# Float32 matmuls in attention and in the product of two weights, heads on row and column halves

## The chip, the cores and the metric

The kernel runs on one core of a Trainium2 chip. The metric is the device time of one execution in microseconds. TensorE (PE) multiplies, VectorE (DVE), ScalarE (ACT) and GpSimd (POOL) compute element by element, SyncE (SP) issues the DMAs. Each engine runs its own instruction stream in order; semaphores order the engines among each other. PEld is the loading of the stationary operand, which overlaps PE.

## The reference

All inputs are float32. Attention over a window of 128 keys, then two gated layers:

```python
batch, n_heads, seq, head_dim = (4, 8, 576, 64)
scores = scale * np.matmul(q, k.transpose(0, 1, 3, 2))
scores = np.where(mask, scores + bias[None], -1000000000.0)   # mask: 0 <= query - key < 128
...
x = np.matmul(attn, v)                    # softmax(scores) @ v, reshaped to 2304 x 512
gate = 1.0 / (1.0 + np.exp(-(x @ w_gate)))
x = gate * (x @ w_val) @ w_out            # 512 -> 1536 -> 512
a = x @ w1
b = x @ w2
h = a * b @ w3                            # 512 -> 1024 -> 1024
out = h @ w_out2                          # -> 512
```

## The kernel before

Every matmul is made of float32r operands. A value is held as a high part (its float32r cast, made on ScalarE) and a low part (value minus high part, on VectorE or POOL), and a product is three matmuls: high x high, high x low, low x high (`product`, L592 to L597). Since `a * b @ w3 @ w_out2` is linear in its last two weights, the kernel multiplies w3 by w_out2 itself, once: 64 products of 128x128 by 128x512 (`fold`, L653), stored to memory and loaded back as the output weight of the second layer.

The tokens go in three passes of 768. A pass has ten groups g of hidden columns, six of the first layer and four of the second. For a group there is a "gate" and a "val" section, each seven products of a fast 2x2 scheme with 384 tokens each (42 matmuls, `multiply`, L675), and mostly a "proj" section (48 matmuls, `project`, L710; "pair0" and "pair1" at the end of a layer). POOL and ScalarE split each group's weights (`weight_sums`, `plain_lo`, `sums_lo`, `out_lo`, L1282 to L1322; `weights_hi`, `out_hi`); VectorE and ScalarE evaluate the results (`keep`, `gate`, `hidden`, `add_up`). At a change of layer the new x is split (`x_hi`, `x_sum`, `x_lo`). Results of a pass stand in `xf` and are stored by `store_pass` (L516), one DMA.

Attention has 80 steps of 128 queries for two heads, grouped in 32 jobs of two or three steps which share loaded keys, queries and values. The keys of a step are one or two chunks of 128 (16 steps have one), 144 chunks in all. A step is: `scores` (L599: head h on rows 64h to 64h+63 of the array, six matmuls), `score` on VectorE (bias, minimum), `exponentials` on ScalarE, `reciprocals` on VectorE, `normalise` on POOL, `turn` on PE (float32 transposes, L622), `turned_hi` on ScalarE and `turned_lo` on VectorE, `pv` on PE (L637, three matmuls a chunk, each 128 columns of values of both heads by 256 columns of probabilities of both heads; the two quarters that pair one head's values with its own probabilities are used) and `out_copy` on ScalarE (L816), one copy per head. Keys, queries and values are split by `keys_hi`, `queries_hi`, `values_hi` (ACT, L769 to L792) and `keys_lo`, `queries_lo`, `values_lo` (POOL, L1232 to L1257).

The first 28 steps (`HEAD`) run ahead of the passes in slots (L730), with lags of 3 to 8 slots between the parts of a step (L69) and two folds per slot; 52 steps run inside the sections of passes 0 and 1, one per section, in the order written for each engine. The PE order in a section is: scores of step n, then the section's products with `turn` of step n-1 after the second and `pv` after the fifth. `scores` waits for the low parts (L603, L604). Two buffer sets for keys, queries and values serve the passes, three the head (`set_of`, L154).

## Time and profile before

| | |
|---|---|
| median of 3 runs | 1037.02 us (1035.7 to 1039.22) |
| profiled execution | 1036.08 us, span 1034.2 us |
| PE busy | 932.4 us, 90% of the span, 5352 matmuls |
| PEld busy | 867.3 us, 84% |
| POOL busy | 736.5 us, 71% |
| ACT busy | 562.4 us, 54% |
| DVE busy | 559.1 us, 54% |
| mean granted PE clock | 0.957 |
| DMA | 80.79 MB, 23.9% of the 16 engines' time |

Busy time of PE counts from the start of a matmul to its modelled end; matmuls overlap, so the distance between two starts, not the duration, is what one costs in a dense stream.

### The profile page before, as it was taken

What the parts mean: (1) busy time and instruction counts of PE and PEld (TensorE: products, weight loads), DVE (VectorE), ACT (ScalarE), POOL (GpSimd) and SP (SyncE); (2) the same over time, 40 slices, a digit from 0 to 9 for tenths busy, and PEclk for the clock granted to TensorE, in tenths of its full rate; (3) what the DMA queues carried; (4) which work ended last, traced back from release to release, by engine and by line L of the source; (5) the groups of instructions that cost most, each with busy time, mean ns of one, the idle gap of its engine ahead of it and who ended that gap; (6) DMA issues with size and microseconds to landing.
All of it is one profiled execution on the core that took longest, in us unless ns stands there. A gap on an engine that the chain in (4) does not pass through costs nothing. (4 is left out here: it accounts for less than half of the span.)

```text
span 1034.2 us, 16072 instructions
## 1 busy us (share of the span) xinstructions
PE 932.4 (90%) x5352; PEld 867.3 (84%) x5352; DVE 559.1 (54%) x1280; ACT 562.4 (54%) x1295; POOL 736.5 (71%) x627
## 2 busy tenths in 40 slices
PE   3988787999997989977999998879987999998998
PEld 2766677999996879976999997869887999997998
DVE  5435353566655556644656655545653755555554
ACT  5867675666674644455666764555443433444340
POOL 4756988777865877758778785788745977658950
PEclk9989898999998989988999999889988999999999
DMA  6335132322121211142221221212103222202201
GB/s 221 113 100 166 45 95 79 98 88 97 48 81 36 69 58 62 51 145 78 82 71 58 87 77 48 86 47 79 62 1 123 68 76 86 78 21 82 82 22 61
DMA packets 46049, 80.79 MB, mean 78 GB/s; under 512 B 4112, under 2 KB 27280, under 8 KB 45968
## 3 DMA queue, kind: packets, MB, share of 16 engines
q1 hardware_dynamic: 45968, 79.77, 23.5%
q8 instruction: 43, 0.70, 0.3%
q14 instruction: 38, 0.31, 0.1%
HBM read 72.94 MB, written 6.82 MB: 77 GB/s over the span
## 5 line engine op out<-in xcount | busy, mean ns | idle before, releaser
L595 PE MATMUL quad_ps<-xs_hi,wq_hi 128*128 128x384 f32 x840 | 299.3, 356 | 23.7 <-ACT sig L866 12.1
L597 PE MATMUL quad_ps<-xs_hi,wq_lo 128*128 128x384 f32 x840 | 289.4, 344 | 0.0
L596 PE MATMUL quad_ps<-xs_lo,wq_hi 128*128 128x384 f32 x840 | 289.2, 344 | 0.0
L595 PEld LDWEIGHTS quad_ps<-xs_hi,wq_hi 128*128 128x128 f32 x840 | 164.4, 196 | 33.1 <-issue 17.0
L595 PE MATMUL o_ps<-h_hi,wo_hi 128*128 128x384 f32 x480 | 168.1, 350 | 11.3 <-DVE xf L1098 10.8
L596 PEld LDWEIGHTS quad_ps<-xs_lo,wq_hi 128*128 128x128 f32 x840 | 164.7, 196 | 0.0
L597 PEld LDWEIGHTS quad_ps<-xs_hi,wq_lo 128*128 128x128 f32 x840 | 163.8, 195 | 0.0
L597 PE MATMUL o_ps<-h_hi,wo_lo 128*128 128x384 f32 x480 | 163.3, 340 | 0.0
L596 PE MATMUL o_ps<-h_lo,wo_hi 128*128 128x384 f32 x480 | 163.0, 340 | 0.0
L1315 POOL TENSOR_TENSOR wq_lo<-wsum,wq_hi 128x1024 fp32r<-128x1024 f32 x60 | 143.7, 2396 | 7.7
L1308 POOL TENSOR_TENSOR wq_lo<-raw_q,wq_hi 128x768 fp32r<-128x768 f32 x60 | 110.8, 1846 | 53.6 <-ACT wq_hi L839 53.6
L1264 POOL TENSOR_TENSOR soft<-soft,recip 128x512 f32<-128x512 f32 (+2 forms) x80 | 75.6, 946 | 80.0 <-DVE recip L1003 79.8
L1048 DVE TENSOR_TENSOR u<-quad_ps,s 128x384 f32<-128x384 f32 x60 | 33.4, 557 | 173.1 <-PE quad_ps L597 171.7
L1098 DVE TENSOR_TENSOR xf<-o_ps,xf 128x384 f32<-128x384 f32 x144 | 79.1, 554 | 69.7 <-PE o_ps L597 68.9
L595 PEld LDWEIGHTS o_ps<-h_hi,wo_hi 128*128 128x128 f32 x480 | 91.4, 190 | 21.1 <-issue 18.7
L872 ACT CAST h_hi<-quad_ps 128x384 fp32r<-128x384 f32 x120 | 57.3, 478 | 87.7 <-DVE quad_ps L1082 87.2
L800 ACT ACTIVATE soft<-soft,negmax 128x256 f32<-128x256 f32 (+2 forms) x160 | 75.0, 471 | 46.7 <-DVE negmax L992 46.5
L596 PEld LDWEIGHTS o_ps<-h_lo,wo_hi 128*128 128x128 f32 x480 | 91.5, 191 | 0.0
L597 PEld LDWEIGHTS o_ps<-h_hi,wo_lo 128*128 128x128 f32 x480 | 91.4, 191 | 0.0
L853 ACT COPY s<-quad_ps 128x384 f32<-128x384 f32 x60 | 28.8, 481 | 108.0 <-PE quad_ps L597 107.8
L1321 POOL TENSOR_TENSOR wo_lo<-wo_lo_raw,wo_hi 128x1024 fp32r<-128x1024 f32 x30 | 71.7, 2391 | 17.6 <-ACT wo_hi L847 17.6
L866 ACT ACTIVATE sig<-quad_ps 128x384 f32<-128x384 f32 x120 | 58.0, 491 | 40.1 <-DVE quad_ps L1071 14.9
(89 smaller groups left out, 1811.0 us busy)
## 6 DMA issues: line engine op xcount, KB each, us to landing
raw_q<-w SPq DMA_DIRECT2D x24, 512.0 KB, 3.5
raw_q<-w_gate SPq DMA_DIRECT2D x18, 512.0 KB, 3.4
raw_q<-w_val SPq DMA_DIRECT2D x18, 512.0 KB, 4.6
wo_lo_raw<-w_out SPq DMA_DIRECT2D x18, 512.0 KB, 3.5
wo_lo_raw<-w_times_wout SPq DMA_DIRECT2D x12, 512.0 KB, 3.6
w_raw<-w3t SPq DMA_DIRECT2D x16, 256.0 KB, 3.4
q_lo_raw<-qT SPq DMA_DIRECT2D x16, 192.0 KB, 3.8
bias<-bias SPq DMA_DIRECT2D x12, 256.0 KB, 4.1
```

The source lines that it names most:

```text
L595: pe.matmul(out, lh, rh, start=start, stop=False, skip_group_check=onto)
L596: pe.matmul(out, lh, rl, start=False, stop=False, skip_group_check=onto)
L597: return pe.matmul(out, ll, rh, start=False, stop=stop, skip_group_check=onto)
L800: op = nc.scalar.activation(cols, cols, ACT.Exp, scale=-1.0, bias=negmax[0:rows, 2 * buf + h:2 * buf + h + 1], accum_out=rowsum[0:rows, 2 ...
L866: nc.scalar.activation(sig[:, piece(blk)], quad[BANK_OUT[blk]][:, 0:TH], func).then_inc(gated, 1)
L872: nc.scalar.copy(h_hi[g % 2][:, piece(blk)], quad[BANK_OUT[blk]][:, 0:TH]).then_inc(h_hi_done, 1)
L1048: nc.vector.tensor_tensor(out=u2[:, :], in0=quad[1][:, 0:TH], in1=s1[:, :], op=ALU.add).then_inc(u2_done, 1)
L1098: op = nc.vector.tensor_tensor(out=xf[:, cols], in0=ps_o[t % 2][:, 0:TH], in1=xf[:, cols], op=ALU.add)
L1264: nc.gpsimd.tensor_tensor(out=cols, in0=cols, in1=recip[0:rows, 2 * buf:2 * buf + 2].unsqueeze(2).to_broadcast([rows, 2, keys.stop - keys. ...
L1308: nc.gpsimd.tensor_tensor(out=wq_lo[m][:, 0:PLAIN], in0=raw_q[m][:, GW:GW + PLAIN], in1=wq_hi[m][:, 0:PLAIN], op=ALU.subtract).then_inc(wq ...
L1315: nc.gpsimd.tensor_tensor(out=wq_lo[m][:, PLAIN:7 * GW], in0=wsum[m][:, :], in1=wq_hi[m][:, PLAIN:7 * GW], op=ALU.subtract).then_inc(wq_sp ...
L1321: nc.gpsimd.tensor_tensor(out=wo_lo[g % 2][:, :], in0=wo_raw[g % 2][:, :], in1=wo_hi[g % 2][:, :], op=ALU.subtract).then_inc(wo_split, 1)
```

## The change

Scores, value product and fold take plain float32 operands: one matmul call where there were three. All casts and subtractions for q, k, v, the probabilities, w3 and w_out2 are dropped, with their buffers and semaphores. In `pv` each head has its own call of 64 weight columns and 128 columns of probabilities, written to its own 64 partitions of the output, so that one `out_copy` of 128 partitions takes both. VectorE copies the turned probabilities (`turned_copy`), in two buffers everywhere. Keys, queries and values have three sets everywhere and are loaded one job earlier in the passes. The head's lags shrink (scores at once, value product four slots later), the folds start at slot 3 instead of 5, and their last 14 come three a slot. The store of a pass is cut into four parts, two of them issued in the last section of the pass and two after the next pass's first loads, with a semaphore for each. Matmuls of the two gated layers, their splits and their order are as before.

```diff
+LAG_NORM, LAG_TURN, LAG_PV = 1, 3, 4
 SLOTS = HEAD + LAG_PV
...
 def fold_slot(k):
-    return 5 + k // 2
+    return 3 + k // 2 if k < 50 else 28 + (k - 50) // 3
...
 FOLDS_IN = [[k for k in range(NFOLD) if fold_slot(k) == s] for s in range(SLOTS + 1)]
...
+W3_LOAD_SLOT = {fold_slot(4 * h - 9): h for h in range(3, HALVES)}
...
-    return j % 3 if j < HEAD_JOBS else j % 2
+    return j % 3
...
+        q_sb = [sb(ctx, f"q_sb{b}", [P, QC], F32) for b in range(3)]
...
+        pt = [sb(ctx, f"pt{b}", [P, 4 * P], F32) for b in range(2)]
...
+            w3_sb = [sb(one, f"w3_sb{k}", [P, IB * P // 2], F32) for k in range(3)]
...
                 if hf >= 3:
-                    w3_half_split(sp, hf - 2)
-                sp.dma_start(w3_raw[hf % 3][:, :], w3t[hf // 2, :, w3_cols(hf)]).then_inc(w3_in[hf % 3], 16)
+                    sp.wait_ge(fold_half, hf - 2)
+                sp.dma_start(w3_sb[hf % 3][:, :], w3t[hf // 2, :, w3_cols(hf)]).then_inc(w3_in[hf % 3], 16)
...
-            def store_pass(p):
...
-                sp.wait_ge(acc_done, tiles_to((p + 1) * GP - 1))
-                sp.dma_start(out_v[:, :, p * TP:(p + 1) * TP],
...
+            def store_part(p, o):
...
+                last = tiles_to((p + 1) * GP - 1) - 8
+                sp.wait_ge(acc_done, last + 1 + max(k for k, (_, part) in enumerate(O_TILES) if part == o))
+                start = o * 2 * TP + p % 2 * TP
+                sp.dma_start(out_v[:, o, p * TP:(p + 1) * TP], xf[:, start:start + TP]).then_inc(out_stored[o], 16)
...
+            load_w3(0)
             load_wo2(0)
-            load_v(0)
             load_wo2(1)
             sp.dma_start(eye[:, :], ident).then_inc(eye_in, 16)
-            load_w3(0)
+            load_k(1)
+            load_q(1)
             load_wo2(2)
-            load_k(1)
             load_wo2(3)
-            load_q(1)
+            load_v(0)
             load_w3(1)
-            load_w3(2)
             load_wo2(4)
             load_wo2(5)
-            load_v(1)
             load_k(2)
             load_q(2)
             load_wo2(6)
             load_wo2(7)
+            load_w3(2)
+            load_v(1)
             load_v(2)
...
-                for j in range(3, HEAD_JOBS + 1):
-                    if s == FIRST[j - 2] + LAG_QK:
+                for j in range(3, HEAD_JOBS + 2):
+                    if s == FIRST[j - 2]:
                         load_k(j)
                         load_q(j)
                     if s == FIRST[j - 2] + LAG_PV:
...
-                if s == 22:
+                if s == 16:
...
             for sec, (g, kind) in enumerate(SECTIONS):
                 if kind == "gate":
-                    if g and g % GP == 0:
-                        store_pass(g // GP - 1)
                     if g + 1 < NG:
                         load_quad(g + 1, 0)
                     load_out(g)
                 if kind == "val" and g + 1 < NG:
                     load_quad(g + 1, 1)
-                for j in range(HEAD_JOBS + 1, len(JOBS)):
-                    if sec == section_of(j - 1):
+                for j in range(HEAD_JOBS + 2, len(JOBS)):
+                    if sec == section_of(j - 2):
                         load_k(j)
                         load_q(j)
-                    if sec == section_of(j - 1) + 1:
+                    if sec == section_of(j - 2) + 1:
                         load_v(j)
+                if kind == "pair1" and g % GP == GP - 1 and g + 1 < NG:
+                    store_part(g // GP, 0)
+                    store_part(g // GP, 1)
+                if kind == "gate" and g and g % GP == 0:
+                    store_part(g // GP - 1, 2)
+                    store_part(g // GP - 1, 3)
...
                 if i == 0:
-                    pe.wait_ge(k_split, j + 1)
-                    pe.wait_ge(q_split, j + 1)
+                    pe.wait_ge(k_in[st], 16 * loads_to(j))
+                    pe.wait_ge(q_in[st], 16 * loads_to(j))
...
-                sides = ((q_hi, k_hi), (q_hi, k_lo), (q_lo, k_hi))
-                for t, (left, right) in enumerate(sides):
-                    for h in range(2):
-                        rows = slice(h * D, (h + 1) * D)
-                        mm = pe.matmul(score_bank(n, h)[:, keys], left[st][rows, q], right[st][rows, where],
-                                       start=t == 0, stop=t == 2)
+                for h in range(2):
+                    rows = slice(h * D, (h + 1) * D)
+                    mm = pe.matmul(score_bank(n, h)[:, keys], q_sb[st][rows, q], k_sb[st][rows, where],
+                                   start=True, stop=True)
                 mm.then_inc(qk_done, 1)
...
             def pv(n):
...
-                    pe.wait_ge(v_split, j + 1)
-                pe.wait_ge(pt_split, n + 1)
+                    pe.wait_ge(v_in[st], 16 * value_loads_to(j))
...
                 for c in chunks_of(n):
                     rows = slice(0, rows_of(n) if c == 1 else P)
-                    vc = slice(key_chunk(n, c) * P, (key_chunk(n, c) + 1) * P)
-                    pc = slice(c * 2 * P, (c + 1) * 2 * P)
-                    mm = product(pv_bank(n)[:, 0:2 * P], (v_hi[st][rows, vc], v_lo[st][rows, vc]),
-                                 (pt_hi[buf][rows, pc], pt_lo[buf][rows, pc]),
-                                 start=c == chunks_of(n)[0], stop=c == 1)
+                    for h in range(2):
+                        left = key_chunk(n, c) * P + h * D
+                        right = (c * 2 + h) * P
+                        mm = pe.matmul(pv_bank(n)[h * D:(h + 1) * D, 0:P], v_sb[st][rows, left:left + D],
+                                       pt[n % 2][rows, right:right + P], start=c == chunks_of(n)[0], stop=c == 1)
                 mm.then_inc(pv_done, 1)
...
             def fold(k):
...
                 if r % 4 == 0:
-                    w3_half_split(pe, k // 4 + 1)
+                    pe.wait_ge(w3_in[hf % 3], 16 * (hf // 3 + 1))
                 if m == 0:
-                    pe.wait_ge(wo2_split, r + 1)
+                    pe.wait_ge(wo2_in[r], 16)
...
-                mm = product(ps_o[m % 2][:, 0:DM], (w3_hi[:, r * P:(r + 1) * P], w3_lo[:, r * P:(r + 1) * P]),
-                             (wo2_hi[:, r * DM:(r + 1) * DM], wo2_lo[:, r * DM:(r + 1) * DM]),
-                             start=r == 0, stop=r == IB - 1)
+                mm = pe.matmul(ps_o[m % 2][:, 0:DM], w3_sb[hf % 3][:, r % 4 * P:(r % 4 + 1) * P],
+                               wo2_sb[:, r * DM:(r + 1) * DM], start=r == 0, stop=r == IB - 1)
...
-                if 0 <= s - LAG_QK < HEAD:
-                    scores(s - LAG_QK)
+                if s < HEAD:
+                    scores(s)
...
-            def turned_hi(n):
-                act.wait_ge(turned, n + 1)
-                wait(act, pv_done, n - 1 if n < HEAD else n)
-                cols = pt_cols(n)
-                nc.scalar.copy(cols(pt_hi[pt_of(n)]), cols(turn_bank(n))).then_inc(pt_hi_done, 1)
...
             def out_copy(n):
...
-                if n >= STEPS_TO[2]:
-                    act.wait_ge(out_stored, 16)
-                rows = rows_of(n)
-                for h in range(2):
-                    op = nc.scalar.copy(out_cols(n, h), pv_bank(n)[h * D:(h + 1) * D, h * P:h * P + rows])
-                op.then_inc(x_ready, 1)
+                if n >= STEPS_TO[2] and n in UNIT_FIRST:
+                    act.wait_ge(out_stored[unit_of(n) % HP], 16)
+                nc.scalar.copy(out_cols(n), pv_bank(n)[:, 0:rows_of(n)]).then_inc(x_ready, 1)
...
+            for s in range(SLOTS + 1):
+                if 0 <= s - LAG_PV - 1 < HEAD:
+                    out_copy(s - LAG_PV - 1)
+                if 0 <= s - 1 < HEAD:
+                    exponentials(s - 1)
...
+            def turned_copy(n):
...
-                dve.wait_ge(pt_hi_done, n + 1)
-                nc.vector.tensor_tensor(out=cols(pt_lo[pt_of(n)]), in0=cols(turn_bank(n)), in1=cols(pt_hi[pt_of(n)]),
-                                        op=ALU.subtract).then_inc(pt_split, 1)
+                dve.wait_ge(turned, n + 1)
+                wait(dve, pv_done, n - 1)
+                nc.vector.tensor_copy(cols(pt[n % 2]), cols(turn_bank(n))).then_inc(pt_done, 1)
...
+            for s in range(SLOTS + 1):
+                if 0 <= s - LAG_TURN < HEAD:
+                    turned_copy(s - LAG_TURN)
+                if s in COPY_SLOT:
+                    fold_copy(COPY_SLOT[s])
                 if 0 <= s - LAG_NORM < HEAD:
                     reciprocals(s - LAG_NORM)
-                if 0 <= s - LAG_TURN - 1 < HEAD:
-                    turned_lo(s - LAG_TURN - 1)
-                if s in COPY_SLOT:
-                    fold_copy(COPY_SLOT[s])
...
+                if s < HEAD:
+                    score(s)
...
-            def keys_lo(j):
-                st, m = set_of(j), key_count(j)
-                pool.wait_ge(k_hi_done, j + 1)
-                nc.gpsimd.tensor_tensor(out=k_lo[st][:, 0:m], in0=k_raw[st][:, 0:m], in1=k_hi[st][:, 0:m],
-                                        op=ALU.subtract).then_inc(k_split, 1)
```

## Rows read from the trace of the kernel before

**Rows 1.** Busy time per stretch, core 0: us, each engine's busy, clock, DMA share, GB/s

```profile
0.00:134.47 134.47, 106.16 (x606) 80.83 (x607) 58.68 (x203) 93.88 (x304) 87.49 (x102) 0.95 0.39 124
134.47:446.12 311.65, 285.79 (x1680) 269.71 (x1678) 180.30 (x401) 182.68 (x395) 239.99 (x191) 0.97 0.22 72
446.12:782.63 336.51, 302.62 (x1750) 284.05 (x1749) 183.33 (x426) 190.75 (x443) 242.14 (x211) 0.93 0.22 71
782.63:1034.20 251.57, 237.85 (x1321) 232.74 (x1320) 136.75 (x253) 95.14 (x155) 166.90 (x125) 0.98 0.21 72
```

**Rows 2.** The same view: gate, val and proj with attention, and without

```profile
223.15:251.70 28.55, 28.44 (x178) 26.79 (x177) 17.30 (x44) 19.28 (x44) 21.79 (x20) 1.00 0.27 91
...
829.37:852.53 23.16, 23.16 (x134) 22.91 (x133) 13.53 (x26) 9.12 (x15) 17.28 (x15) 1.00 0.21 69
```

**Rows 3.** Timeline of PE: start us, duration us, line, tiles, shapes, count

```profile
17.46 0.80 PE L595 MATMUL o_ps<-wo_hi,w_hi 128*128 128x512 f32 x1 [3.87 <-POOL w_lo L1350]
...
30.62 0.60 PE L633 MATMUL quad_ps<-eye,soft 128*128 128x128 f32 x4
...
67.95 0.39 PE L595 MATMUL o_ps<-wo_hi,w_hi 128*128 128x512 f32 x1
68.18 0.39 PE L596 MATMUL o_ps<-wo_lo,w_hi 128*128 128x512 f32 x1
...
68.95 0.28 PE L618 MATMUL quad_ps<-k_lo,q_hi 64*128 64x256 f32 x2
69.07 0.28 PE L618 MATMUL quad_ps<-k_hi,q_lo 64*128 64x256 f32 x2
69.28 0.39 PE L595 MATMUL attn_ps<-pt_hi,v_hi 128*128 128x256 f32 x1
```

**Rows 4.** Timeline of POOL and PE where the second hole ends

```profile
365.92 0.99 POOL L1243 TENSOR_TENSOR q_lo<-q_lo_raw,q_hi 128x384 fp32r<-128x384 f32 x1
...
367.01 0.47 PE L618 MATMUL attn_ps<-k_hi,q_hi 64*128 64x128 f32 x2 [5.06 <-issue]
```

**Rows 5.** Busy time in the four holes, then in four stretches behind them

```profile
168.60:172.65 4.05, 0.12 (x3) 0.04 (x2) 0.57 (x1) 0.69 (x2) 3.97 (x6) 1.00 0.56 216
361.80:367.01 5.21, 0.15 (x1) 0.03 (x1) 0.57 (x1) 0.73 (x2) 5.13 (x8) 0.75 0.49 153
470.30:477.50 7.20, 0.00 (x1) 0.03 (x1) 1.49 (x3) 2.28 (x4) 7.12 (x9) 0.73 0.53 182
678.80:684.41 5.61, 0.17 (x1) 0.03 (x1) 0.57 (x1) 0.74 (x2) 5.53 (x9) 0.77 0.50 164
...
173.00:176.50 3.50, 3.50 (x15) 3.43 (x14) 0.51 (x4) 1.12 (x2) 3.50 (x4) 0.54 0.00 0
364.30:371.20 6.90, 4.19 (x16) 4.10 (x17) 0.51 (x4) 1.03 (x4) 6.90 (x7) 0.51 0.08 28
477.50:484.00 6.50, 6.50 (x25) 6.29 (x26) 2.00 (x7) 2.60 (x9) 6.36 (x4) 0.51 0.01 3
681.80:688.70 6.90, 4.29 (x17) 4.10 (x18) 0.78 (x4) 1.03 (x4) 6.90 (x8) 0.51 0.23 86
```

**Rows 6.** What PE waited for: us in total, times, longest us

```profile
PE quad_ps L595 <- ACT sig L866: 12.1, 3, 5.2
...
PE o_ps L595 <- POOL w_lo L1350: 10.0, 5, 3.9
...
PE quad_ps L618 <- POOL q_lo L1243: 8.5, 1, 8.5
```

**Rows 7.** Timeline of SP and ACT where the third pass starts

```profile
783.42 0.40 SPq L519 DMA_DIRECT2D outT<-xf  x1
...
784.40 1.01 SPq L506 DMA_DIRECT2D wo_lo_raw<-w_out  x1
...
792.34 1.04 ACT L847 CAST wo_hi<-wo_lo_raw 128x1024 fp32r<-128x1024 f32 x1 [7.99 <-DMA wo_lo_raw<-w_out]
```

**Rows 8.** Groups by line: shapes, count, busy us, mean ns, idle before

```profile
L1010 DVE TENSOR_TENSOR pt_lo<-attn_ps,pt_hi 128x512 fp32r<-128x512 f32 x36 | 24.6, 683 | 3.4 <-ACT pt_hi L814 3.2
```

235 lines of the change are left out of this document (41 added, 194 removed).

## The prediction

> **What bounds the kernel now.** I read the stages first: busy time of every engine in four stretches of the span [rows 1]. The first, 0 to 134.47 us, is the head: the first 28 of 80 attention steps, interleaved with the folding product. The other three are the three passes, from each pass's first product to the next one's. In the last pass, which has no attention, TensorE (PE) is busy 94.5% at a clock of 0.98; in the head it is 79% (106.16 of 134.47), in the first two passes 92% and 90%, at clocks of 0.97 and 0.93. The second reading is a quiet stretch with attention against one without, each a gate, a val and a proj section [rows 2]: 28.55 against 23.16 us, so a step costs 1.80 us of TensorE where nothing waits, the other engines below 80%. 52 such steps on the 23.16 us rate do not explain the passes, so the third reading is the waits of TensorE and the stretches in which they lie. Four times TensorE stands still 4 to 7 us at the start of a step [rows 5]; twice it waits over 5 us for the sigmoid (two of the three waits behind the 12.1 us in [rows 6]). TensorE is the bound, but with some 60 us of holes and of half clock behind the holes. So the change must be priced in two currencies: what it adds to TensorE's own stream, and which holes it closes.
>
> **The clock.** In the stretch 364.30 to 371.20 us, from the middle of one of the four holes on, the granted clock is 0.51, the lower of the two levels (1.2 against 2.4 GHz) [rows 5]. TensorE resumes at 367.01 [rows 4] and so works about 4.2 us at half rate, which costs 2.1 us. The rows behind the other three holes read 0.54, 0.51 and 0.51 as well [rows 5], with 3.5, 6.5 and (from 684.4) 4.3 us of work in them: 18.5 us at half rate, 9 lost.
>
> **Part 1: one float32 matmul for three of float32r.** No float32 product is in the trace; only float32 transposes are. The rows show the pace of the float32r passes at full clock [rows 3]: 0.23 us per pass of 512 columns, 0.12 per 256 columns (score passes; the value product's have as many columns and I price them the same); and the two heads of a score start together (one entry, x2), so a pair of 64-row passes costs one pass. Float32 lower bound: one pass, like the transposes, of which four take 0.60 us, at most 0.15 each for 128 columns [rows 3]. Value taken: the kernel writes each number as two parts and leaves out low times low; a product which keeps everything has four partial products for its three, so I take four passes at the float32r pace. Upper bound: four passes per head with no overlap at all.
> By that row of transposes alone a float32 operand costs one pass. The Trainium skill (FP8 and Floating Point Precision, TensorE Precision Notes) says that true float32 takes four passes through the array. By the skill the folds cost 0.92 us each, by the row 0.23; the row is of a transposition, where nothing is summed, and I do not lean on it.
>
> Folding: 64 products, 3 x 0.23 = 0.69 before, 4 x 0.23 = 0.92 after: +14.7 us, all in the head, where folds are the largest item and hide behind nothing.
>
> Scores: before, h0 and h1 alternate pass by pass, so three pairs cost 3 x 0.12 = 0.36. After, each head is one call; its passes come one behind the other on the same rows of the array, and the next head can start only when the earlier head's last part is running. I take half overlap: two parts of two passes for each head, the second of one beside the first of the other, three units of two passes, 6 x 0.12 = 0.72: +0.36 per step. Full overlap would be 4 x 0.12 = 0.48 (+0.12), none 8 x 0.12 = 0.96 (+0.60). 80 steps: +29, of it 10 in the head.
>
> Value product: before, three passes of 256 columns with 128 weight columns, half of the result thrown away: 0.36 per chunk of 128 keys, 144 chunks. After, 128 columns per head, 64 weight columns, one head on each column half. A pass of 128 columns is taken as 0.06, half of the 256 row (nearest rows with 128 columns: the transposes at 0.15 or less, loading 128 weight columns each). With the same half overlap, two chunks are five units of 0.12, 0.30 per chunk: -0.06. Full overlap 0.24 (-0.12), none 0.48 (+0.12). Sum -9, of it -3 in the head.
> Changing blocks costs already: the last score pass starts at 69.07 and the next value pass at 69.28, 0.21 instead of 0.12 [rows 3]. The Trainium skill (TensorEngine Tiling, Key Properties) states that changing the tiling mode drains the engine, which speaks against column halves between full-width work. By it a step gets one or two drains more; at the 0.1 of the row that is 8 to 16 us over 80 steps; by the rows alone it is nothing, as value products already stand behind transposes of another shape. I keep it in the range, not in the sum.
>
> Transposes are unchanged. Turned probabilities: a cast on ScalarE goes and VectorE's subtraction (683 ns) becomes a copy of the same size out of PSUM [rows 8]; I price the copy at the same 0.68. The turn-to-value chain is shorter by the cast, but other products of TensorE stand between and hide it: nothing. New waits: VectorE's copy waits for the transposes themselves (before: for the cast behind them) and for the value product of the step before; behind it on VectorE are the reciprocals of the next step and, in the head, the next `score`. Both events lie a section or a slot's first microsecond back, so I price them at nothing; were the value product late, the next scores would pay the 0.68 of the copy. The one output copy instead of two on ScalarE: nothing, same cover.
>
> **Part 2: holes that close in the passes.** The scores of a job wait for POOL's low parts of keys and queries. POOL makes the last of these from 365.92 to 366.91; TensorE's scores start at 367.01 [rows 4]. All four holes have this form: 4.05, 5.21, 7.20 and 5.61 us, POOL busy 98% in each [rows 5]: 22.1 us. Afterwards scores wait for the load alone, issued one job earlier with three buffer sets. The holes' clock goes too: 9 us. What is late next: POOL's low parts of the next section's weights (L1308, L1315), which stand in its queue behind what it does in the hole, and ScalarE's copy of the first product, queued behind a cast that waits for POOL's sums (L841). POOL is relieved of three subtractions of about 1 us per job (the row of queries: 0.99 [rows 4]), so it nearly holds the pace; I give back 4 us over the four places, an estimate, 1 us each.
>
> Stores: the pass's output leaves as one transfer issued on SP ahead of the loads (783.42, L519); the w_out load behind it (784.40) frees ScalarE's cast only at 792.34 [rows 7], and the sigmoid and TensorE behind it. Afterwards two parts are issued before and two behind the loads, each with its own semaphore; the load needs no wait for the last sum. Price: 5.3 + 5.2 us of the 12.1 [rows 6], plus about 4 us of half clock. Behind the last two store parts SP has only loads for later sections (a bias, the next weights), and their wait ends with the last sum, a few us into the gate section: nothing.
>
> Fewer POOL operations also shift the x splits at the changes of layer forward; TensorE waits there for VectorE and for the copy of the first product. I take 3 us.
> Passes: scores +19, value -6, holes -22.1 - 9 + 4, stores -10.5 - 4, the rest -3: about -32.
>
> **Part 3: the head.** Added: 14.7 + 10 - 3 = +22. Removed: waits for the low part of w3, 10.0 us in five [rows 6]; the first scores waited 8.5 us for the split queries [rows 6] and need the load alone, about 2 us sooner; the first fold, at 17.46 [rows 3], follows the third step instead of the fifth and no longer two splits: 2 more than the wait already counted; waits for POOL's normalisation, 4 (behind splits in its queue); clock: 0.95 over 134.47 us is 6.7 lost [rows 1], half comes back: 3.4. That is -22. So the head stays as long as it is, bound more by TensorE: 0. The loads of w3 now wait until eight products earlier are done, 4 slots of 3.5 to 4 us ahead: hidden.
>
> **Sum.** The profiled execution took 1036.1 (span 1034.2, 1.9 around it), 0.9 under the median of 1037.0. 1036.1 + 0 - 32 = 1004; I write 1003.
>
> **Rivals.** (A) Full overlap of the two heads: 80 x (-0.24) and 144 x (-0.06), 28 us less: 975. For it: heads start together in the rows. Against it: they alternate there, which the new order of calls does not. (B) The holes come back as waits for the weights' low parts: half of the 45 us of Part 2: about 1025. For it: POOL is busy 77% in the first pass and 72% in the second [rows 1]. (C) Slower: no overlap between the heads. Scores +0.24 and value +0.18 x 1.8 chunks over the forecast, 0.56 per step: +45, 1048; it decides when a score takes over 0.86 instead of 0.72 per step with a like excess in the value product. (D) Slower: float32 work leaves the clock at 1.2 GHz in the head, where all of TensorE's work is then float32. Some 100 us of work at half rate: 1100. Nothing in the rows speaks for it but that no float32 product is among them. (E) One pass per float32 product: folds 0.46 less than before each, then the steps' own chain bounds the head: about 955. (F) The change does not do what it says: the compiled products equal three passes each: scores and folds as before, holes closed: 967, counted with A.
>
> **Chances.** Forecast 0.42, A with F 0.25, B 0.12, C 0.09, D 0.07, E 0.05. The forecast's own range is 985 to 1022 (drains up, overlap down). A, B and E are faster; the upper edge of B and the lower of C touch 1037. Within 0.3% is about what can be told from no change. Faster 0.82, same 0.04, slower 0.14. Range: 962 to 1036 leaves out D, most of C and E.
>
> **What would show it.** A fold's matmul pace of 0.92 per product; a score block of 0.72 and a value chunk of 0.30; no PE wait over 2 us at a score; the ScalarE cast of wo at a pass's start right behind its predecessors; first product of the passes near 134; 28.55 for gate, val and proj becoming about 29.3. The prediction is wrong if a score block takes as long as 0.48 or 0.96, if POOL holds PE at the weights in four places, or if the clock row of the head falls below 0.9.

## The result, and the profile after

The changed kernel takes 957.8 us in the median of four runs (953.7 to 959.1), against 1036.5 for the kernel before on the same chip: a ratio of 0.923, 95% interval 0.920 to 0.926. The forecast was 1003, its range 962 to 1036. The direction was right, and the gain was more than twice the one forecast. The profiled execution of the changed kernel took 958.4 us, span 956.7.

The stages again, busy time of each engine in the head and the three passes (columns as in [rows 1]):

```profile
0.00:113.55 113.55, 105.02 (x533) 50.95 (x533) 50.40 (x186) 50.35 (x181) 42.45 (x49) 1.00 0.48 152
113.55:407.37 293.82, 282.64 (x1679) 254.67 (x1677) 176.52 (x399) 151.98 (x320) 212.59 (x166) 0.99 0.25 80
407.37:710.79 303.42, 292.04 (x1745) 259.52 (x1745) 179.84 (x426) 157.68 (x345) 211.40 (x169) 0.99 0.23 76
710.79:956.70 245.91, 236.54 (x1321) 230.95 (x1320) 136.51 (x253) 95.46 (x155) 166.73 (x125) 0.99 0.21 68
```

Against [rows 1] the head is 20.9 us shorter (forecast: 0), the passes 17.8, 33.1 and 5.7, together 56.6 (forecast: 32). In the head TensorE is busy about as long as before, 105.0 against 106.2, so 19.8 of the 20.9 us that went there are standing still: 28.3 us before, 8.5 now. In the passes it stands still 41.5 us less (73.5 before, 31.9 now) and is busy 15.0 us less. The clock stands at 0.99 or 1.00 everywhere, where the four stages read 0.95, 0.97, 0.93 and 0.98.

A quiet stretch with attention beside one without, as in [rows 2] (gate, val and proj of group 3 and of group 22):

```profile
193.39:222.17 28.78, 28.78 (x175) 25.63 (x174) 17.30 (x44) 16.15 (x35) 18.81 (x17) 1.00 0.25 85
750.77:773.93 23.16, 23.16 (x134) 22.91 (x133) 13.51 (x26) 9.11 (x15) 17.62 (x15) 1.00 0.19 69
```

28.78 where 29.3 was forecast and 28.55 (28.44 of it busy) stood before; the part without attention is the same to the hundredth. So nothing was won in the quiet work: the 57 us of the passes are holes (stretches in which TensorE stands still), other waits and clock.

The timeline of TensorE in the middle of the head (start, duration, line, tiles, shapes, count; L628 is the fold, L583 the scores, L615 the value product, L598 the transposes). A block is a run of such matmuls of one kind, and its price is the time from its first start to the next block's first start:

```profile
60.40 1.88 PE L628 MATMUL o_ps<-wo_sb,w_sb 128*128 128x512 f32 x4
62.21 0.70 PE L583 MATMUL quad_ps<-k_sb,q_sb 64*128 64x256 f32 x4
62.84 0.44 PE L615 MATMUL attn_ps<-pt,v_sb 128*64 128x128 f32 x4
63.22 0.65 PE L598 MATMUL quad_ps<-eye,soft 128*128 128x128 f32 x4
```

A float32 call shows as two matmuls: two folds are x4 and take 1.81 us to the next start, 0.90 each. Inside the block the matmuls start 0.43 us apart, so a float32 call costs 0.86 there, 3.7 times the 0.23 of a float32r pass over as many columns. The Trainium skill (FP8 and Floating Point Precision, TensorE Precision Notes) gives true float32 four passes, and the trace agrees: taken as four, they are 0.21 us each. A score block over 256 keys takes 0.63 to the next start, a value product over one chunk 0.37, over two 0.59 (medians). In the kernel before the same blocks took 0.55 for scores, 0.74 (in the passes) to 0.82 (in the head) for two chunks, 1.57 for two folds.

Around the value product of the passes the price does not end with the block. The neighbours, full-width matmuls of 384 columns, start 0.17 us apart among themselves. Before the change the value product had their tile shape; first that, then the column halves:

```profile
229.28 0.34 PE L597 MATMUL quad_ps<-xs_hi,wq_lo 128*128 128x384 f32 x1
229.46 0.31 PE L595 MATMUL attn_ps<-pt_hi,v_hi 128*128 128x256 f32 x1
...
230.20 0.34 PE L595 MATMUL quad_ps<-xs_hi,wq_hi 128*128 128x384 f32 x1
230.37 0.34 PE L596 MATMUL quad_ps<-xs_lo,wq_hi 128*128 128x384 f32 x1
```

```profile
199.62 0.34 PE L564 MATMUL quad_ps<-xs_hi,wq_lo 128*128 128x384 f32 x1
199.88 0.66 PE L615 MATMUL attn_ps<-pt,v_sb 128*64 128x128 f32 x8
200.47 0.44 PE L562 MATMUL quad_ps<-xs_hi,wq_hi 128*128 128x384 f32 x1
200.75 0.34 PE L563 MATMUL quad_ps<-xs_lo,wq_hi 128*128 128x384 f32 x1
```

The block is 0.15 us shorter, but it starts 0.09 later behind its neighbour, and the second matmul behind it 0.10 later. From the last matmul ahead to the second behind, the median for two full chunks is 1.09 us before and 1.14 after, for one chunk 0.71 and 0.92, for two of which the second has 64 keys 1.44 and 1.28.

What TensorE waits for now (us in total, times, longest):

```profile
PE quad_ps L562 <- ACT s L783: 9.8, 7, 3.7
PE o_ps L562 <- DVE xf L988: 7.3, 10, 2.0
PE attn_ps L598 <- DVE negmax L882: 6.7, 2, 3.3
PE quad_ps L583 <- DMA q_sb<-qT: 5.6, 1, 5.6
```

The three rows of [rows 6] are gone: the low parts of w3 and of the queries do not exist, and the wait for the sigmoid is 0.5 in one. The 5.6 is the first load of queries, at the start. The start of the third pass, where [rows 7] had the store ahead of the load:

```profile
710.99 0.34 SPq L468 DMA_DIRECT2D wo_lo_raw<-w_out  x1
711.37 0.91 SPq L483 DMA_DIRECT2D outT<-xf  x2
...
715.11 1.05 ACT L777 CAST wo_hi<-wo_lo_raw 128x1024 fp32r<-128x1024 f32 x1 [2.59 <-DMA wo_lo_raw<-w_out]
```

The cast starts 4.1 us after the load's issue instead of 7.9. And the copy that took the place of the subtraction in [rows 8] (L901, 680 ns against 683) is as long as that, as priced.

### The profile page after: what moved, and what is told of

It reads as the page before. It is cut to its first block and busy times, and to the rows that moved or that the text cites. A ratio compares the mean times of both kernels' runs of the same rounds, so it can differ in the third digit from the quotient of the medians.

```text
span 956.7 us, 15336 instructions
## 1 busy us (share of the span) xinstructions
PE 916.2 (96%) x5272; PEld 796.1 (83%) x5272; DVE 543.3 (57%) x1261; ACT 455.5 (48%) x999; POOL 633.2 (66%) x507
## 5 line engine op out<-in xcount | busy, mean ns | idle before, releaser
L564 PE MATMUL quad_ps<-xs_hi,wq_lo 128*128 128x384 f32 x840 | 283.9, 338 | 0.0
L563 PE MATMUL quad_ps<-xs_lo,wq_hi 128*128 128x384 f32 x840 | 283.7, 338 | 0.0
L562 PEld LDWEIGHTS quad_ps<-xs_hi,wq_hi 128*128 128x128 f32 x840 | 159.7, 190 | 32.5 <-issue 18.8
L563 PEld LDWEIGHTS quad_ps<-xs_lo,wq_hi 128*128 128x128 f32 x840 | 159.9, 190 | 0.0
L564 PEld LDWEIGHTS quad_ps<-xs_hi,wq_lo 128*128 128x128 f32 x840 | 159.6, 190 | 0.0
L977 DVE TENSOR_TENSOR h_lo<-quad_ps,h_hi 128x384 fp32r<-128x384 f32 x120 | 65.9, 549 | 19.9 <-ACT h_hi L802 18.6
```

Of the source, the lines that this page charges most:

```text
L562: pe.matmul(out, lh, rh, start=start, stop=False, skip_group_check=onto)
L563: pe.matmul(out, lh, rl, start=False, stop=False, skip_group_check=onto)
L564: return pe.matmul(out, ll, rh, start=False, stop=stop, skip_group_check=onto)
L977: nc.vector.tensor_tensor(out=h_lo[g % 2][:, piece(blk)], in0=quad[BANK_OUT[blk]][:, 0:TH], in1=h_hi[g % 2][:, piece(blk)], op=ALU.subtrac ...
```

## The experiments

Names with "b_" start from the kernel before and take parts of the change; those with "a_" start from the changed kernel. Times are medians; ratios are to the kernel before on the same chip (1036.5 beside the changed kernel, 1037 to 1038 beside the others). "First product" is the start of the first full product of the passes, the end of the head.

| kernel | us | ratio, 95% | first product |
|---|---|---|---|
| before | 1036.5 | | 134.5 |
| after | 957.8 | 0.920 to 0.926 | 113.6 |
| b_scores32 | 992.1 | 0.955 to 0.959 | 122.5 |
| b_values32 | 1004.6 | 0.967 to 0.971 | 115.3 |
| b_att32 | 969.0 | 0.933 to 0.936 | 108.9 |
| b_fold32 | 1028.3 | 0.989 to 0.993 | 125.6 |
| b_both32 | 974.2 | 0.937 to 0.941 | 113.0 |
| b_store | 1025.3 | 0.987 to 0.990 | 135.1 |
| b_att32s | 956.2 | 0.920 to 0.923 | 109.2 |
| a_store | 969.5 | 0.934 to 0.937 | 112.8 |
| a_fold3 | 963.4 | 0.928 to 0.931 | 118.3 |
| a_onehalf | 1012.0 | 0.974 to 0.978 | 133.8 |
| a_full | 970.9 | 0.934 to 0.938 | 122.2 |
| a_poolwait | 986.2 | 0.949 to 0.953 | 114.8 |
| a_pool | 964.3 | 0.926 to 0.934 | 112.7 |
| a_order | 945.0 | 0.910 to 0.913 | 113.9 |
| b_att32so | 944.1 | 0.909 to 0.913 | 109.1 |

**Which part of the change does it.**

b_att32: attention alone.

```
-                    pe.wait_ge(k_split, j + 1)          (and q_split, v_split)
+                    pe.wait_ge(k_in[st], 16 * loads_to(j))
...
```

The rest of the edit, in words: the three float32r passes of scores and value product, the casts on ScalarE and the subtractions on POOL go; one float32 matmul for each head (in the value product, for each head and chunk) reads q_raw, k_raw and v_raw; VectorE copies the turned probabilities, and the outputs lie on column halves.

> The kernel before (1036) with attention alone on float32 operands, heads on row and column halves: the casts and subtractions of queries, keys, values and turned probabilities are gone. Order, lags, two buffer sets after the head, loads one job ahead, the whole pass's store and the folding product are those of before. By the blocks of the two traces a step's scores cost 0.09 more and its value product 0.15 less, so TensorE's own stream hardly moves; what is to be seen is whether the four holes close without the third buffer set and the earlier loads. Theory that POOL's subtractions alone made the holes: -22 for the holes and -9 for their clock, some -10 for the value products and what waits fall in the head: 990 to 1000, no wait over 2 us at a score. Rival, the load itself comes late with one job's lead: two or more of the four holes stay, 1010 to 1020.

969.0: 68 of the 79 us, below the range of the theory, and more than I had given the whole change. No wait of TensorE for keys, queries or values is left behind the first load, with loads one job ahead and two buffer sets. The waits of its head:

```profile
PE quad_ps L614 <- DMA q_lo_raw<-qT: 5.2, 1, 5.2
PE quad_ps L614 <- DVE negmax L964: 5.2, 1, 5.2
PE o_ps L593 <- POOL w_lo L1314: 2.7, 1, 2.7
```

The wait for w3's low part went from 10.0 [rows 6] to 2.7 us although the fold was not touched.

b_scores32 and b_values32 take the two halves of that edit one at a time.

> The kernel before (1037) with the scores alone on float32: no casts and subtractions of queries and keys, scores wait for the loads. Values, turned probabilities and all else as before. By the blocks TensorE pays 80 x 0.09 = +7. If the prediction's part is right, the four holes (22.1) and their clock (9) go, and the first scores come 3 us sooner: about 1037 + 7 - 22 - 9 + 4 - 3 = 1014; if the scores' splits also made the waits of the head and the x sums behind POOL: 985 to 1000.

> The kernel before (1037) with the value product alone on float32 column halves: no casts and subtractions of values and of turned probabilities, those of queries and keys as before. By the blocks TensorE saves 0.15 us per pair of chunks and 0.09 per single chunk, some 11 in all, in the prediction 9: 1026 with all four holes still there. Rival, ScalarE and POOL get the room and queries' low parts come in time: at least two holes gone, 1005 or less.

The scores give 45.4, the values 32.9; together they would be 78, and they share 10. The scores' part closes the four holes and gives 22 us more than the prediction's terms do (992 against 1014): it is the second case of its expectation. The values' part leaves the holes where they were, as expected, and still gives three times its price: TensorE's waits at the scores of the passes are still

```profile
PE attn_ps L616 <- issue: 12.8, 4, 6.8
```

but its head is 19.2 us shorter, where the blocks of the value product explain some 6. The stage row of that head, against the first of [rows 1]:

```profile
0.00:115.32 115.32, 95.89 (x655) 67.81 (x655) 58.57 (x203) 80.81 (x256) 75.05 (x82) 0.99 0.46 144
```

ScalarE has 13 us less to do and POOL 12, TensorE stands still 19.4 us instead of 28.3, and its clock is 0.99 instead of 0.95. Length times what the clock lacks to 1 is 6.7 us before and 1.2 here, so some 5 of the 19 are clock.

b_fold32: the folding product alone on float32; b_both32: this and attention.

```
-                mm = product(ps_o[m % 2][:, 0:DM], (w3_hi..., w3_lo...), (wo2_hi..., wo2_lo...), ...)
+                mm = pe.matmul(ps_o[m % 2][:, 0:DM], w3_raw[k // 4 % 3][:, ...], wo2_raw[:, ...], ...)
```

> The kernel before (1036) with the folding product alone on float32: no cast, no subtraction of w3 and w_out, TensorE waits for the loads. All else as before. By the prediction's sum the fold costs 14.7 us more (10.9 by the pace of 0.858 us that the changed kernel shows), and the waits for w3's low part (10), the first fold (2) and half the head's clock (3.4) go: 1032 to 1036, head still near 134. Rival, the casts and subtractions of the fold held up the whole chain of the head (ScalarE and POOL do them ahead of the exponentials and the normalisation), and with them the 21 us that the head lost: 1015 to 1020, head near 115.

> The kernel before with attention and the folding product on float32, old lags, loads, buffer sets and the one store. Against attention alone (969.0): if the fold's float32 costs its passes, 64 x 0.12 to 0.17, and only the wait of 2.7 us for w3's low part and a first fold some 3 us earlier come back, 972 to 974; rival, additive with the fold alone on the kernel before (-8.7): 960.

Alone it gives 9, between the two theories; on top of attention it costs 5 (974.2 against 969.0, intervals apart). In the heads of these two kernels, TensorE's busy time and clock:

```profile
0.00:108.93 108.93, 94.63 (x597) 63.13 (x597) 55.47 (x200) 72.00 (x230) 53.20 (x56) 1.00 0.49 153
```

```profile
0.00:112.99 112.99, 104.74 (x533) 50.38 (x533) 43.64 (x185) 59.03 (x208) 41.97 (x49) 1.00 0.46 147
```

The first is b_att32, the second b_both32: 10.1 us more of busy TensorE against 6.1 less of standing still. By the blocks, two folds take 1.55 us in b_att32 and 1.81 in b_both32, 32 x 0.26 = 8.4, and the transposes ahead of them 0.08 more, 28 x 0.08 = 2.2: the 10 us again.

a_fold3: in the changed kernel the fold as three float32r passes again.

```
+W3_HI_SLOT = {fold_slot(4 * h) - 2: h for h in range(HALVES)}
+W3_LO_SLOT = {fold_slot(4 * h) - 1: h for h in range(HALVES)}
+                mm = product(ps_o[m % 2][:, 0:DM], (w3_hi[hf % NW3][:, w], w3_lo[hf % NW3][:, w]), ...)
```

> The changed kernel (958) with the folding product alone as three float32r passes again: w3 and w_out cast on ScalarE two slots ahead of their use, subtracted on VectorE (w_out, every second half of w3) and POOL one slot ahead, three buffers each for the high and the low halves of w3; all else, slots of the folds too, as in the changed kernel. Theory: with attention's casts and subtractions gone, ScalarE (17 of 40 us busy from 20 to 60) and POOL (10 of 40) have room, and the fold costs TensorE 0.12 to 0.17 us less per product, 64 x 0.12 = 8: 950, head near 106. Rival: the waits for the low parts of w3 (10 us in the kernel before) come back and the first fold waits for the casts: 958 to 965.

963.4: the rival. The changed kernel's slots leave the splits no time:

```profile
PE o_ps L577 <- POOL w_lo L1219: 7.4, 6, 4.3
```

TensorE waits 2.4 us more for the low parts that VectorE makes, and the first fold stands at 15.9 instead of 11.8. With the old lags (b_att32) the same form is the fastest of all heads, 108.9. Three float32r passes need the lead; one float32 call does not.

**The stores.** a_store puts the one transfer back; b_store makes the edit alone.

```
+                    if g and g % GP == 0:
+                        store_pass(g // GP - 1)
                     if g + 1 < NG:
                         load_quad(g + 1, 0)
                     load_out(g)
```

> The changed kernel (958) with the pass's output stored as one transfer ahead of the loads of the next pass's first weights, as before the change, and one semaphore for it. Prediction's price for that part: 10.5 us of waits for the sigmoid and 4 of half clock, 972. Rival by the sections of the two traces: the gate and val sections at the starts of passes two and three took 14.0, 5.4 and 2.8 us less, 22 in all, 980. Rival, other work hides it once POOL has fewer subtractions: under 962.

> The kernel before with the stores in four parts and nothing else changed. Prediction's price: 10.5 us of waits for the sigmoid and 4 of half clock, 1022.6. In the changed kernel the same edit is worth 11.5 us: 1025.6. Rival: POOL's subtractions, a hole of their own in these sections, take the place of the store: within 5 us of 1037.

11.7 and 12.4 us (b_store as expected from a_store): the part is nearly independent of the rest. The 14.5 was some 3 too much, and the 22 that I read off the sections of the two traces afterwards was nearly twice too much: one of these sections held one of the four holes too. In a_store the cast for the third pass again waits 8 us for a load issued behind the store (the store's issue stands at 717.39):

```profile
718.38 1.01 SPq L468 DMA_DIRECT2D wo_lo_raw<-w_out  x1
...
726.31 1.04 ACT L773 CAST wo_hi<-wo_lo_raw 128x1024 fp32r<-128x1024 f32 x1 [7.98 <-DMA wo_lo_raw<-w_out]
```

b_att32s is b_att32 with the stores in four parts.

> The kernel before with two parts of the change only: attention on float32 (969.0 by itself) and the stores in four parts. Order, lags, two buffer sets and the folding product in float32r as before. If the stores are worth 11.5 here as in the changed kernel: 957.5, no slower than the whole change (958), so that the folding product on float32 and the new lags and loads together bring nothing. Rival, the rest of the change is worth 5 us or more: 963 or above.

956.2: level with the whole change. Attention and stores are the change; the fold on float32, the third buffer set, the loads two jobs ahead and the new lags bring nothing together that can be told from none.

**Do the heads overlap.** a_onehalf puts both heads on one row half and one column half, a_full the value product on the full width.

```
-                    rows = slice(h * D, (h + 1) * D)
+                    rows = slice(0, D)
-                        mm = pe.matmul(pv_bank(n)[h * D:(h + 1) * D, 0:P], v_sb..., pt...)
+                        mm = pe.matmul(pv_bank(n)[0:D, 0:P], v_sb..., pt...)
```

> The changed kernel (958 us) with both heads' scores on rows 0 to 63 of the array and both heads' value products on columns 0 to 63, so that the two heads of a step can no longer run beside each other. Head 1's scores are those of head 0, and both heads' value products are summed in the place of head 0. Same numbers of products, columns, loads and waits (one more small copy on ScalarE per step). Theory of full overlap: in the changed kernel a score block takes 0.63 us and a pair of value chunks 0.59 us because the two heads share their time; without it a score block gets some 4 x 0.107 = 0.43 longer (80 steps: +34) and a chunk of the value product, four passes of 128 columns at a fourth of 0.107 x 2 each, 0.2 longer (144 chunks: +29): about 1015 to 1025. Rival, little overlap to lose (a float32 product is cheap by itself, its passes short): under +10, so below 968.

1012.0, +54, just under the 1015 to 1025 of full overlap and far from the rival's 968. Blocks of its timeline: two chunks of values at 62.30, the second with 64 keys, take 1.15 us to the transposes at 63.45 (0.74 in the changed kernel; two full chunks take 1.02 against 0.59), and scores over 128 keys 0.64; over 256 keys the median is 1.06:

```profile
61.66 0.71 PE L583 MATMUL quad_ps<-k_sb,q_sb 64*128 64x128 f32 x4
62.30 1.23 PE L615 MATMUL attn_ps<-pt,v_sb 128*64 128x128 f32 x8
63.45 0.44 PE L598 MATMUL quad_ps<-eye,soft 128*128 128x128 f32 x2
```

1.06 against 0.63 is the whole of the second head's four passes, 4 x 0.107. So the overlap in the changed kernel is full, not half, although each head is one call.

> The changed kernel with the value product over the full width: one float32 call per chunk of keys, 128 weight columns against the 256 columns of both heads, half of the result thrown away as before the change, and two output copies on ScalarE. Scores and folds as changed. Theory: four passes of 256 columns at 0.107 us are 0.43 per chunk instead of the 0.21 which a chunk takes with both heads side by side, 144 x 0.21 = +30: 988, a pair of chunks at 1.0 instead of 0.59. Rival, the column halves bring drains that full width saves: under +20, below 978.

```
+                    mm = pe.matmul(pv_bank(n)[:, 0:2 * P], v_sb[st][rows, left:left + P],
+                                   pt[n % 2][rows, right:right + 2 * P], ...)
```

970.9, +13 where I expected +30: the rival. In the head the price is near what I worked out, 8.6 us over 28 steps (48 chunks at 0.21 would be 10); in the passes a quiet gate section grows from 9.37 to 9.47 only. There the value product lies between full-width matmuls, and on the full width it is one of them:

```profile
238.37 0.34 PE L564 MATMUL quad_ps<-xs_hi,wq_lo 128*128 128x384 f32 x1
238.55 1.05 PE L613 MATMUL attn_ps<-pt,v_sb 128*128 128x256 f32 x4
239.24 0.53 PE L562 MATMUL quad_ps<-xs_hi,wq_hi 128*128 128x384 f32 x1
239.61 0.34 PE L563 MATMUL quad_ps<-xs_lo,wq_hi 128*128 128x384 f32 x1
```

From the last matmul ahead to the second behind it takes 1.24 us, against 1.14 on column halves. That is nearly what its eight passes through the array come to: two neighbours at 0.17 and eight times 256 columns at 0.107 are 1.20. On column halves the same sum is 0.34 + 0.43 = 0.77, and 0.37 us more goes at the changes of shape: 0.09 ahead, 0.10 behind, the rest inside the block. Over one chunk the full width is even the cheaper, 0.78 against 0.92. The Trainium skill (TensorEngine Tiling, Key Properties) has a drain at a change of tiling, and these rows agree that such a change costs time. Of the 0.37 the kernel before did not pay the 0.19 outside the block: over the 52 steps of the passes that is 10 us, inside the 8 to 16 that the prediction kept in its range and left out of its sum.

**What made the four holes.** POOL's subtractions of keys, queries and values back in the changed kernel, waited for (a_poolwait) or not (a_pool):

```
+                        nc.gpsimd.tensor_tensor(out=k_part[...], in0=k_sb[st][...], in1=k_sb[st][...], op=ALU.subtract)
+                        nc.gpsimd.tensor_tensor(out=q_part[...], ...).then_inc(parted, 1)   (v_part alike)
+                    wait(pe, parted, j - HEAD_JOBS)          (a_poolwait only)
```

> The changed kernel with POOL's three subtractions per job of passes one and two put back where they stood (keys and queries one section ahead of the job's scores, values in its first section), into tiles of their own that nothing reads; TensorE's scores and value products wait for them. No casts. Tile sets, loads and order as changed. Theory that POOL's queue made the four holes: POOL gets some 3 us per job more and the holes come back at a score, 3 to 6 us each, 980 to 990. Rival, it was the casts on ScalarE ahead of the subtractions: POOL keeps up, under 965.

> The same as the run with POOL's subtractions put back and waited for, but TensorE waits for none of them. If the holes came from POOL's load alone, which then delays the low parts of the weights (rival B of the prediction), this costs as much as the waited form, 975 or more; if they came from the wait, it stays within 5 us of the changed kernel.

986.2 and 964.3 (960.6 to 969.4). Waited for, four holes are back, of 5.2, 5.2, 3.2 and 3.0 us, in the same sections as before (groups 1, 7, 10, 17) and in the same form as in [rows 4]: POOL ends at 150.19, TensorE starts at 150.40.

```profile
149.37 0.82 POOL L1196 TENSOR_TENSOR q_part<-q_sb 128x384 f32<-128x384 f32 x1
```

```profile
150.40 0.80 PE L590 MATMUL attn_ps<-k_sb,q_sb 64*128 64x128 f32 x4 [5.17 <-issue]
```

Not waited for, the same work on POOL costs 6.5 in the median of runs that spread over 9: a little more than the 5 that I had allowed if the wait made the holes, and far from the 17 or more of rival B. It is the place in POOL's queue in front of which TensorE stands, with the casts of ScalarE not needed for it.

**A version faster than both.** In the changed kernel three holes stand at the change of layer (groups 6, 16, 26), as before the change. The first, on VectorE and TensorE:

```profile
296.20 2.55 DVE L924 TENSOR_TENSOR xt<-xf,xt 128x768 f32<-128x768 f32 x1
298.68 0.41 DVE L882 CUSTOM_DVE_ANT_0 soft<-attn_ps,bias 128x256 f32<-128x256 f32 x1
```

```profile
299.59 1.09 PE L598 MATMUL attn_ps<-eye,soft 128*128 128x128 f32 x4 [3.35 <-DVE negmax L882]
```

TensorE's transposes wait for the next step's scores to leave their bank, and these stand on VectorE behind an x sum that only the last of seven products needs; the copy `s` of the first product waits on ScalarE (until 299.60) behind the cast of that sum. After the hole TensorE runs at 0.52 us instead of 0.33 per product, the clock of 295 to 304 us being 0.69. a_order:

```
                 if n is not None:
                     score(n)
+                if kind == "gate" and g % GP == G1:
+                    x_lo(instance(g), P2)
+                    x_sum(instance(g), P4)
 ...
                 if n is not None:
                     exponentials(n)
+                if kind == "gate" and g % GP == G1:
+                    x_hi(instance(g), P4)
```

> The changed kernel with another order at the change of layer (groups 6, 16, 26): on VectorE the next step's scores stand before the low part of x for P2 and the x sum for P4 instead of behind them, and on ScalarE the cast of that sum stands behind the copy of the first product and the exponentials. Nothing is added or removed. Theory: TensorE's holes of 3.7, 3.7 and 4.1 us at those gate sections (the transposes wait for the scores behind a 2.6 us sum beside POOL's; the copy of the first product waits behind the cast) close, and some 2 us of half clock after each with them: 945 to 950. Rival, the moved sum and the casts behind it hold up P3 and P4 of the same section by as much: within 2 us of 958.

945.0 (944.2 to 947.2), 13 below the change and at the good end of the theory. The same place, VectorE and TensorE:

```profile
295.05 0.41 DVE L886 CUSTOM_DVE_ANT_0 soft<-attn_ps,bias 128x256 f32<-128x256 f32 x1
...
297.13 2.59 DVE L928 TENSOR_TENSOR xt<-xf,xt 128x768 f32<-128x768 f32 x1
```

```profile
297.00 0.60 PE L598 MATMUL attn_ps<-eye,soft 128*128 128x128 f32 x4
```

> The kernel before with attention on float32, the stores in four parts and the reordered change of layer; folding product in three float32r passes, old lags and loads. Attention and stores gave 956.2, the new order 13.0 on the changed kernel: 943. If it is no slower than the reordered changed kernel (945.0), the folding product on float32 and the new schedule of the head bring nothing to the time.

944.1 (942.7 to 945.1): no different from a_order. With this order, too, the fold on float32 and the new schedule of the head together earn nothing and lose nothing.

## Why the prediction was wrong in size

The sum missed by 45 us: the terms of the matmuls by 26 (18 in the head, 8 in the passes), the rest of the passes by 18, the head's removals by 3, with holes and stores nearly even.

**The pace of scores: the step that failed most.** "I take half overlap" made 0.72 for a score, six times 0.12. The records show 0.63 for 256 keys with the change of shape included, 0.43 of it passes: full overlap, rival A, and a_onehalf shows what none would be. The change of shape is no part of the difference, as a score block before the change had it too (0.55, of which I had counted 0.36). And 32 of the 80 steps have fewer than 256 keys, where I priced all alike. The difference per step is +0.08 us for 256 keys, +0.02 for 192 and -0.06 for 128: 3 us over 80 steps instead of 29.

**Value product.** 0.30 per chunk came out (0.29), but by luck: half overlap was wrong here too, and the change of shape that I had left out of the sum made up for it. The 0.36 before was 0.37 to 0.41. By the blocks the term is -14 us, -6 in the head and -7 in the passes; but in the passes the neighbours of the block pay 10 for the changes of shape, which leaves +2 there, and -4 in all instead of -9. **Fold.** 0.90 in its block against 0.78 before: +7.8 instead of +14.7, as I had 0.92 and 0.69; the transposes ahead of it start it 0.08 later (28 steps, +2). The three terms were +35 in the sum and measure +9.

**The head.** "Bound more by TensorE: 0" was right in what bounds it and wrong in the terms: +22 should have been +4, and the -22 of removals was about -25. But I had put the removals to the wrong parts. The 10 us for w3's low part I gave to the fold; b_att32 and b_values32 (10.0 to 2.7 and 3.7) remove most of it with the fold as it was. They take attention's casts out of ScalarE's queue and its subtractions out of POOL's, and the fold's splits stand in both; which of the two queues it was no run divides. "The turn-to-value chain is shorter by the cast, but other products hide it: nothing" is not borne out in the head: b_values32 is 19 us shorter there with some 6 us of blocks and 5 of clock to explain it. How much of the rest is that chain and how much the queues, no run here divides.

**Holes.** The mechanism was right, and the sum too, in part by luck: a_poolwait gives back 28.4 us for my 27.1. The parts differ: 16.6 us of holes and, by length times what the clock lacks, some 13 of clock, where I had 22.1 and 9, less 4. The cure was not the third buffer set and the earlier load, as the part implied: b_att32 has neither. Rival B does not occur (wq_lo holds TensorE for 1.2 us in three).

**Stores.** 14.5 priced, 11.7 and 12.4 measured.

**The rest of the passes: the second step that failed.** I gave 3 us to x splits and nothing else. The passes lost 56.6 us though their matmuls cost 5 more; holes (28) and stores (12) leave 21 of it. By the stage rows 41.5 us are standing still, and the 15.0 of less busy time with the 5 on top are 20 of clock, where I had counted 13 for the passes. One place of the 21 can be seen in the kernel before, in the val section of group 19, on VectorE, POOL and TensorE:

```profile
745.36 5.04 DVE L1034 TENSOR_TENSOR xt<-xf 128x768 f32<-128x768 f32 x1
```

```profile
745.15 2.39 POOL L1321 TENSOR_TENSOR wo_lo<-wo_lo_raw,wo_hi 128x1024 fp32r<-128x1024 f32 x1
747.51 0.72 POOL L1294 TENSOR_TENSOR wsum<-raw_q 128x256 f32<-128x256 f32 x1
748.19 0.72 POOL L1296 TENSOR_TENSOR wsum<-raw_q 128x256 f32<-128x256 f32 x1
748.87 0.72 POOL L1299 TENSOR_TENSOR wsum<-wsum,raw_q 128x256 f32<-128x256 f32 x1
749.66 1.32 POOL L1302 TENSOR_TENSOR wsum<-raw_q,wsum 128x256 f32<-128x256 f32 x1
```

```profile
751.10 1.09 PE L633 MATMUL attn_ps<-eye,soft 128*128 128x128 f32 x4 [3.45 <-DVE negmax L992]
```

VectorE's sum lies beside four POOL operations that stand back to back, and ends 0.7 us after the first pause between two of them (749.59 to 749.66); the operation behind that pause takes 1.32 instead of 0.72. TensorE waits for the scores that stand behind the sum on VectorE. In the changed kernel the same sum takes 1.36 (680.24), and the section 9.20 instead of 15.40 us. The runs tell which part does it: the sum takes 5.0 wherever the values are still split (b_scores32, b_fold32, b_store) and 1.4 in b_values32, where they are not while keys and queries still are. With POOL's subtractions put back in a_pool it takes 3.66, and TensorE waits 2.0 us behind it:

```profile
679.85 3.66 DVE L930 TENSOR_TENSOR xt<-xf 128x768 f32<-128x768 f32 x1
```

The Trainium skill (SBUF — State Buffer, SBUF: two separate sides) calls the port pair that the two engines share an exclusive lock, taken by whichever starts first and held for its whole operation, also against a VectorE operation with two SBUF inputs. The trace agrees that the two hold each other up: the sum takes 0.96 us alone, and POOL's operation beside its end grows by 0.6. How long the loser waits depends on where it starts. Beside the 2.39 us operation VectorE waited for the whole run behind it too; in the changed kernel, where it starts beside the first short one, it got in behind that one, though POOL made no pause. That rule spoke to this change, and I had not weighed it. I had read the waits by their largest rows, and this one stood, as four waits of together 11.2, among those left out. The clock is in the rest too: the length of a stage times what its clock lacks to 1, over the four stages, is 45 us in [rows 1] and 8 in the rows of after, 36 less, part of it in time that TensorE stood still; I had counted 16 of it (9 in the four holes, 4 at the stores, 3.4 in the head). What else makes up the 21 was not traced.

**Rivals.** A was given 975 with F and a quarter; overlap is full as in A, and its three terms, +7, are close to the +9 measured. The time is 17 below A for what A shares with the forecast, the rest of the passes above all. C and D do not occur (a float32 head at clock 1.00). E's time nearly came out, for none of its reason (a fold takes 0.90, not one pass). Of the signs, the fold's 0.92 came near (0.90); the first product near 134 (113.6) and the score block of 0.72 (0.63) did not show.

## What to carry to other kernels

Price a block together with its neighbours, from the last start ahead of it to the second start behind it, before and after alike: the pace inside a block leaves out the change of shape, which cancelled for the scores and ate the whole gain of the value product in the passes. When a change takes work off an engine's queue, look at what else stands in that queue: attention's splits stood with the fold's in the queues of ScalarE and POOL, and most of the wait that the profile booked on w3 went when attention was relieved. Do one part at a time on the kernel before: two of the change's parts gave everything, and a further 13 us lay in an order that the change had left alone.

## What the runs showed of the hardware

Two float32 calls on the two row halves run fully beside each other though each call is two matmuls: 0.63 us for a pair over 256 keys, 1.06 on one half (a_onehalf). Taken as four passes, float32 goes at 0.21 us per pass over 512 columns, where a float32r pass over as many takes 0.23 [rows 3]. A value product on column halves between full-width matmuls takes 0.37 us more than its passes and its neighbours' (1.14 against 0.77), on the full width 0.04 more (1.24 against 1.20). An x sum on VectorE with both inputs in SBUF takes 0.96 us by itself and 5.04 where it starts beside a subtraction of 2.39 us on POOL with three short operations behind it, back to back; without the values' subtractions ahead of these on POOL it takes 1.36, with POOL's subtractions put back 3.66 (a_pool). That it is the shared port is the Trainium skill's reading; the rows show the two engines' times.
